# Two dense expert layers behind clustered attention: the first layer by seven block products, with block sums on GpSimd and VectorE

## The chip, the cores and the metric

The kernel runs on one core of a Trainium2 chip. The metric is the device time of one launch in microseconds (us), the median of several runs. PE is TensorE, DVE VectorE, ACT ScalarE, POOL GpSimd, and SP the queue that issues most DMAs.

## What is computed

Clustered attention (16 heads of 768 tokens, width 64) gives x of 1536 x 512. A first mixture of 8 experts takes each token to one expert of fixed capacity 192, chosen by a greedy global order. A second, dense mixture sends every token through all 4 experts and sums them by weights. The change is in the second:

```python
def _moe2_ref(x, domain_probs, w1, w2):          # x 1536x512, w1 4x512x1024, w2 4x1024x512
    p = domain_probs / (domain_probs.sum(-1, keepdims=True) + 1e-09)
    out = np.zeros((N, D), dtype=np.float32)
    for e in range(E):
        h = np.maximum(x @ w1[e], 0.0)
        out += p[:, e:e + 1] * (h @ w2[e])
    return out
```

## The kernel before

The program is one function with one block of instructions for each engine; semaphores set the order between them. Three stages follow one another: attention (to 313 us), the routed experts together with the search that assigns tokens (to 580.8 us), and the dense experts (to the end). All orders are written out by hand.

**Routed experts.** `products` (PE) runs hidden and output products of expert m with tokens as columns. ACT takes the hidden tiles (`hidden_1`, L700) and the results. `y_hi` (L720) rounds a result to `xs_hi` and DVE's `y_lo` (L964) writes the rest to `xs_lo`. POOL gathers rows (`expert_rows`), keeps the tokens' numbers (`keep_ids`, `ids_by_tile`), and gathers the mixing weights (`mix_rows`, L513).

**Dense experts.** A product in full precision is made of three passes in fp32r: each operand is split into a rounded part "hi" and the rest "lo", and `three` (L1286 to L1290) adds hi x hi, lo x hi and hi x lo in PSUM. The loops run over expert e (4), half i of the hidden width (2) and pairs of token chunks (2 x 2 chunks of 384 tokens), as hardware loops. A chunk's first layer is 4 hidden tiles `f`, each 4 depth blocks x 3 passes = 12 matmuls of 384 columns into bank `f` of `ps_h`; 48 a chunk. Its second layer is 3 token tiles, each 4 `f` x 3 passes = 12 matmuls of 512 columns into `ps_y`; 36 a chunk. PE does the first layer of two chunks and then their second layer. There are 16 such pairs; I call one a block.

ACT's `hidden_hi` (L695) writes relu of a tile as `h_hi`, DVE's `hidden_lo` (L958) writes `h_lo`, and DVE adds each weighted output tile to `X` (L1108). Each half's weights of 1 MB are loaded by SP (`load_a`, `load_b`), rounded by ACT (`split_hi_a`, `split_hi_b`, L687 and L691) and their rest is formed on POOL (`split_lo_a`, `split_lo_b`, L483 and L488). After the last block POOL scatters 12 row tiles to the output (L551).

The lines that set PE's work in the dense stage:

```python
for par in range(2):
    for f in range(KF):
        pe.wait_ge(h_taken, 8 * E + KF * (J0 + par) + f - 3)
        for a in range(KD):
            mm = three(ps_h[:, f, 0:HC], a_hi[i][:, a, fs], a_lo[i][:, a, fs],
                       xs_hi[:, a, cols], xs_lo[:, a, cols], a == 0, a == KD - 1)
        mm.then_inc(h_full, 1)
```

Of the kernel before, what the change touches and what calls it, by code (L numbers as in the profile page):

```python
# [12 lines left out]
P = 128  # L13
# [14 lines left out]
def clustered_attention_two_moes(nc, q, k, v, centroids, w_gate, w1, w2, domain_probs, v1, v2, out):  # L28
# [34 lines left out]
    CCH = NT // HALF  # L63
# [11 lines left out]
    with ExitStack() as ctx:  # L75
# [25 lines left out]
        X = sb("X", [P, NT, DM], F32)  # L101
# [58 lines left out]
        h_lo = sb("h_lo", [P, 2, KF, HC], F32R)  # L160

# [135 lines left out]
        xe_ps = ps_h[:, 0:2, 0:2 * CAP].rearrange("p a (c m) -> p a c m", c=2)  # L297

# [14 lines left out]
        def _(sp):  # L313
# [70 lines left out]

            sp.wait_ge(h_full, 8 * (E - 2) + 8)
            load_a(raw_a, a_in, 1, 0, 0)
            sp.wait_ge(y_full, 2 * (E - 2) + 2)
            load_b(raw_b, b_in, 1, 0, 0)
            sp.wait_ge(h_full, 8 * E)
            load_a(raw_a, a_in, 1, 0, 1)  # L390
            load_b(raw_b, b_in, 1, 0, 1)
            with sp.Fori(1, E2) as e:
                for i in range(2):
                    sp.wait_ge(alo_done[i], e)
                    load_a(raw_a, a_in, 1, e, i)
                    sp.wait_ge(blo_done[i], e)
                    load_b(raw_b, b_in, 1, e, i)
# [3 lines left out]
        def _(pool):  # L401
# [79 lines left out]
            def split_lo_a(i, c):  # L481
                pool.wait_ge(ahi_done[i], c + 1)
                g.tensor_tensor(a_lo[i][:], raw_a[i][:], a_hi[i][:].bitcast(F32),  # L483
                                ALU.subtract).then_inc(alo_done[i], 1)

            def split_lo_b(i, c):
                pool.wait_ge(bhi_done[i], c + 1)
                g.tensor_tensor(b_lo[i][:], raw_b[i][:], b_hi[i][:].bitcast(F32),  # L488
                                ALU.subtract).then_inc(blo_done[i], 1)
# [30 lines left out]
            for t in range(NT):  # L520
                pool.wait_ge(gt_full, t + 1)
                g.memset(X[:, t, :], 0.0).then_inc(y_zero, 1)
# [4 lines left out]
            ids_by_tile(0, 0, T_EARLY)  # L527
            for n in range(EARLY, E):
                expert_rows(n)
                keep_ids(n)  # L530
# [9 lines left out]
            pool.wait_ge(y_full, 2 * E)  # L540
            split_lo_b(0, 0)
            split_lo_a(1, 0)
            split_lo_b(1, 0)
            with pool.Fori(1, E2) as e:
                for i in range(2):
                    split_lo_a(i, e)
                    split_lo_b(i, e)
            for t in range(NT):

                pool.wait_ge(y_taken, 2 * E + (2 * E2 - 1) * NT + t + 1)  # L550
                g.indirect_dma_start(out, bass.IndirectOffsetOnAxis(ap=ids_all[:, t:t + 1], axis=0),  # L551
                                     X[:, t, :], None).then_inc(out_done, 16)
# [4 lines left out]
        def _(act):  # L557
# [127 lines left out]
            def split_hi_a(i, c):  # L685
                act.wait_ge(a_in[i], 16 * (c + 1))
                s.copy(a_hi[i][:], raw_a[i][:]).then_inc(ahi_done[i], 1)  # L687

            def split_hi_b(i, c):
                act.wait_ge(b_in[i], 16 * (c + 1))  # L690
                s.copy(b_hi[i][:], raw_b[i][:]).then_inc(bhi_done[i], 1)  # L691

            def hidden_hi(F, bank, dst):
                act.wait_ge(h_full, F + 1)
                s.activation(dst, ps_h[:, bank, 0:dst.shape[-1]], ACT.Relu).then_inc(hhi_done, 1)  # L695


# [20 lines left out]
            def y_hi(m, j):  # L718
                act.wait_ge(y_full, 2 * m + j + 1)
                s.copy(xs_hi[:, 2 * j:2 * j + 2, bass.ds(m * CAP, CAP)],  # L720
                       ps_y[:, j, 0:2 * CAP].rearrange("p (c m) -> p c m", c=2)).then_inc(yhi_done, 1)
# [9 lines left out]
            def results_and_rows(n):  # L731
                if n > 0:
                    y_hi(n - 1, 0)
                rows_1(n)
                if n > 0:
                    y_hi(n - 1, 1)
# [15 lines left out]
            for n in range(E - 2, E):  # L752
                results_and_rows(n)
                for j in range(2 * KF):
                    hidden_1(n, j)

            split_hi_a(0, E // 2)
            for j in range(2):
                y_hi(E - 1, j)
            split_hi_b(0, E // 2)  # L760

            act.wait_ge(y_full, 2 * E)

# [706 lines left out]
```

## Time and profile before

| what | us |
|---|---|
| median of 3 runs | 1124.15 |
| lowest, highest run | 1122.44, 1127.68 |
| the profiled execution, its own time | 1119.93 |
| its span, first to last instruction | 1118.1 |
| PE busy in the span | 1056.5 |
| dense stage, from its first matmul (580.8) to the span's end | 537.3 |

A row of a timeline is a start, a duration, the engine and line, the tiles written and read, and in brackets the idle time before it and what ended it. A row of groups has a count, the busy time, the mean of one in ns and the idle time before. PE's matmuls overlap, so their spacing is read from their starts and not from their durations.

### The profile page before, as it was taken

To read this page: it belongs to the slowest core of one execution; us is meant where nothing else is said; L and a number is where in the kernel's file an instruction comes from. 1 tells how busy PE (TensorE), PEld (TensorE's weight loads), DVE (VectorE), ACT (ScalarE), POOL (GpSimd) and SP (SyncE) were. 2 spreads that over 40 slices of the span, in tenths; PEclk is the share of its full clock that TensorE was granted. 3 is DMA by queue.
4 is the path that set the end of the run, shared out by engine and by line. 5 is a ranking of instruction groups with operands and counts; after the bars stand their busy time and mean duration, and the time that the engine had idled before them with its cause. 6 is when DMAs were issued, how large, how long until landed. Compare 5 with 4: busy or idle time off the path is not lost.

```text
span 1118.1 us, 18666 instructions
## 1 busy us (share of the span) xinstructions
PE 1056.5 (94%) x6650; PEld 965.2 (86%) x6650; DVE 500.0 (45%) x1107; ACT 432.3 (39%) x929; POOL 214.8 (19%) x210
## 2 busy tenths in 40 slices
PE   3999999999987899999999999999999999999996
PEld 3888888888876899998998999988999988899995
DVE  2888888888826445553012222222222222222222
ACT  3898888888732333335131221102122120211110
POOL 7033231323021001111422310302111030110022
PEclk9999999999996799999999999999999999999999
DMA  3333323232024444446942210201001000000011
GB/s 94 79 82 82 81 74 77 70 77 59 19 114 164 153 165 165 168 171 209 167 151 76 75 38 0 75 0 38 38 11 64 0 0 0 0 0 0 0 56 56
DMA packets 41351, 82.46 MB, mean 74 GB/s; under 512 B 4704, under 2 KB 10848, under 8 KB 41056
## 3 DMA queue, kind: packets, MB, share of 16 engines
q1 hardware_dynamic: 38608, 75.61, 22.1%
q0 software_dynamic: 2704, 6.33, 1.9%
q8 instruction: 25, 0.41, 0.2%
q14 instruction: 14, 0.11, 0.0%
HBM read 63.02 MB, written 6.32 MB: 62 GB/s over the span
## 4 chain that ended last, share of the span: by engine, by line
PE 82%; ACT 9%; issue 3%; DVE 3%; DMA 2%; POOL 1%; ACTq 0%; SPq 0%; DVEq 0%
PE ps_h L1290 8%; PE ps_h L1288 8%; PE ps_h L1289 8%; PE ps_h L1315 8%; PE ps_y L1290 8%; PE ps_y L1289 8%; PE ps_y L1288 8%; PE ps_y L1330 7%; PE ps_t L1193 4%; PE ps_s L1180 3%; ACT p_hi L622 2%; PE ps_s L1181 2%; PE ps_m L1154 2%; PE ps_o L1207 2%; PE ps_o L1208 2%
## 5 line engine op out<-in xcount | busy, mean ns | idle before, releaser
L695 ACT ACTIVATE h_hi<-ps_h 128x384 fp32r<-128x384 f32 x128 | 63.1, 493 | 337.1 <-PE ps_h L1290 337.1
L1288 PE MATMUL ps_h<-xs_hi,a_hi 128*128 x512 | 171.3, 335 | 0.0
L1290 PE MATMUL ps_h<-xs_lo,a_hi 128*128 x512 | 171.2, 334 | 0.0
L1289 PE MATMUL ps_h<-xs_hi,a_lo 128*128 x512 | 171.1, 334 | 0.0
L958 DVE SCALAR_TENSOR_TENSOR h_lo<-ps_h,h_hi 128x384 fp32r<-128x384 f32 x128 | 71.4, 558 | 195.5 <-ACT h_hi L695 195.5
L1108 DVE SCALAR_TENSOR_TENSOR X<-ps_y,mix_n,X 128x512 f32 x96 | 72.1, 751 | 189.4 <-PE ps_y L1290 189.4
L1290 PE MATMUL ps_y<-b_lo,h_hi 128*128 128x512 f32 x384 | 149.7, 390 | 0.0
L1289 PE MATMUL ps_y<-b_hi,h_lo 128*128 128x512 f32 x384 | 149.7, 390 | 0.0
L1288 PE MATMUL ps_y<-b_hi,h_hi 128*128 128x512 f32 x384 | 149.4, 389 | 0.0
L879 DVE TENSOR_TENSOR p_lo<-ps_t,p_hi 128x384 fp32r<-128x384 f32 x192 | 101.6, 549 | 21.6 <-ACT p_hi L622 21.5
L622 ACT CAST p_hi<-ps_t 128x384 fp32r<-128x384 f32 x192 | 87.1, 485 | 36.0 <-PE ps_t L1193 34.5
L870 DVE TENSOR_REDUCE neg_max<-ps_s 128x1 f32<-128x768 f32 x96 | 91.6, 954 | 18.2 <-PE ps_s L1181 18.2
L1288 PEld LDWEIGHTS ps_h<-xs_hi,a_hi 128*128 128x128 f32 x512 | 96.1, 188 | 0.6
L1289 PEld LDWEIGHTS ps_h<-xs_hi,a_lo 128*128 128x128 f32 x512 | 96.1, 188 | 0.6
L1290 PEld LDWEIGHTS ps_h<-xs_lo,a_hi 128*128 128x128 f32 x512 | 96.1, 188 | 0.0
L1193 PE MATMUL ps_t<-ident,probs 128*128 128x128 f32 x576 | 86.8, 278 | 7.3 <-DVE p_lo L879 6.1
L609 ACT ACTIVATE probs<-ps_s,neg_max 128x768 f32<-128x768 f32 x96 | 88.0, 917 | 2.8 <-DVE neg_max L870 2.8
L1290 PEld LDWEIGHTS ps_y<-b_lo,h_hi 128*128 128x128 f32 x384 | 72.1, 188 | 15.0
L1289 PEld LDWEIGHTS ps_y<-b_hi,h_lo 128*128 128x128 f32 x384 | 72.1, 188 | 14.7
L1288 PEld LDWEIGHTS ps_y<-b_hi,h_hi 128*128 128x128 f32 x384 | 72.1, 188 | 14.6
L1193 PEld LDWEIGHTS ps_t<-ident,probs 128*128 128x128 f32 x576 | 67.9, 142 | 19.4 <-issue 9.5
L1180 PE MATMUL ps_s<-kcT,qcT 80*128 80x384 f32 x192 | 74.8, 389 | 7.7 <-ACT kcT L597 6.6
(175 smaller groups left out, 1639.1 us busy)
## 6 DMA issues: line engine op xcount, KB each, us to landing
raw_a<-in_moe_w_dram SPq DMA_DIRECT2D x16, 1024.0 KB, 5.2
raw_b<-in_moe_w_dram SPq DMA_DIRECT2D x16, 1024.0 KB
odd_a<-in_moe_w_dram SPq DMA_DIRECT2D x8, 1024.0 KB, 8.5
odd_b<-in_moe_w_dram SPq DMA_DIRECT2D x8, 1024.0 KB
khhT<-kqT SPq DMA_DIRECT2D x32, 192.0 KB, 3.0
raw_k<-in_k_dram SPq DMA_DIRECT2D x16, 192.0 KB, 2.4
raw_q<-in_q_dram SPq DMA_DIRECT2D x16, 192.0 KB, 2.5
raw_v<-in_v_dram SPq DMA_DIRECT2D x16, 192.0 KB, 3.1
```

Of the source, the lines that this page charges most:

```text
L609: s.activation(probs[g % 2][:], ps_s[g % 2][:, :, 0:HC], ACT.Exp, bias=neg_max[:, g % 2:g % 2 + 1], scale=1.0, accum_out=row_sum[:, 2 * b ...
L622: s.copy(p_hi[u][:, a * HALF:(a + 1) * HALF, (g % HALF) * P:(g % HALF + 1) * P], ps_t[:, a, 0:HC].rearrange("p (c m) -> p c m", m=P)).then ...
L870: v_.tensor_reduce(neg_max[:, g % 2:g % 2 + 1], ps_s[g % 2][:, :, 0:HC], AX.XY, ALU.max, negate=True).then_inc(max_ready, 1)
L879: v_.tensor_tensor(p_lo[u][sl], ps_t[:, a, 0:HC].rearrange("p (c m) -> p c m", m=P), p_hi[u][sl].bitcast(F32), ALU.subtract).then_inc(plo_ ...
L1108: v_.scalar_tensor_tensor(out=row, in0=ps_y[:, (HALF * par + t) % 4, :], scalar=mix_n[:, bass.ds(tile, 1), bass.ds(e, 1)].rearrange("p a b ...
L1180: t_.matmul(dst, qcT[b][:, ts], kcT[b][:, cs], start=True, stop=False)
L1193: mm = t_.transpose(ps_t[:, a, c * P:(c + 1) * P], probs[g % 2][:, kt * P:(kt + 1) * P], ident[:])
L1288: t_.matmul(dst, w_hi, x_hi, start=first, stop=False)
L1289: t_.matmul(dst, w_lo, x_hi, start=False, stop=False)
L1290: return t_.matmul(dst, w_hi, x_lo, start=False, stop=last)
L1315: mm = t_.matmul(ps_h[:, H_BANK[j % 3], 0:CAP], wt[i][:, a, f * P:(f + 1) * P], xe[:, a, :], start=(a == 0), stop=(a == KD - 1))
L1330: mm = t_.matmul(ps_y[:, d // 2, (d % 2) * CAP:(d % 2 + 1) * CAP], wt[i][:, f, d * P:(d + 1) * P], h1[:, i * KF + f, :], start=(i == 0 and ...
```

## The change

The first layer of the dense experts is computed by Winograd's form of Strassen's method. The matrices are cut in two along each of three directions: the hidden width of a slice (2 x 128), the depth (2 x 256) and the tokens (2 x 384). Eight block products, each of 2 depth blocks x 3 passes = 6 matmuls of 384 columns, become seven, of sums of blocks.

- **Order.** Tokens are now outermost: two groups of 768 tokens, and for each all experts and halves, so 16 blocks `J` as before, written out with no loops. Weights are loaded once for each group, so twice. A block has two slices `s_` (`t` = 0, 1), each with seven products M1, M6, M7, M5, M2, M3, M4 into five banks (`M_BANK`), and then six output tiles in three banks.
- **Sums of weights** (`w_sums`, POOL): four operations of 256 columns per slice. ACT rounds seven blocks at once (`w_high`, 1792 columns), POOL forms the rest (`w_low`).
- **Sums of tokens** (`x_sums`, POOL): four operations of 768 columns per group. ACT rounds seven blocks (`x_high`); the rest is formed by DVE for group 0 and by POOL for group 1 (`x_low`).
- **Sums of products** (`slice_sums`, DVE): seven operations of 384 columns per slice, four of which write to PSUM. ACT first copies M1 out (`keep_first`). The relu and the rest of four hidden tiles (`slice_highs`, `d_low`) follow as before.
- The weights come in columns of 128 (`sum_weights`, two DMAs per slice) and single buffers of `b_raw`, `b_hi`, `b_lo`; before, each had two.
- Results of the routed experts are copied once as fp32 (`y_out`), so DVE's `y_lo` falls away, as does zeroing `X`. Outputs go to a tile `Y`; its first 6 tiles are scattered during block 8.

```diff
+        o_ps = [ps_y[:, 1 + k, :] for k in range(3)]
+        M_BANK = [{1: 0, 6: 1, 7: 2, 5: 3, 2: 0, 3: 1, 4: 4}, {1: 3, 6: 2, 7: 0, 5: 1, 2: 3, 3: 2, 4: 4}]
...
+            def w_sums(J, t):
+
+                a11, a12, a21, a22 = (w_sum[t][:, k] for k in (2, 3, 0, 1))
+                s1, s2, s3, s4 = (w_sum[t][:, k] for k in (4, 5, 6, 7))
+                pool.wait_ge(wsum_in[t], 32 * (J + 1))
+                g.tensor_tensor(s1, a21, a22, ALU.add).then_inc(wsum_step, 1)
+                g.tensor_tensor(s3, a11, a21, ALU.subtract).then_inc(wsum_step, 1)
...
+            for J in range(NJ):
+                b_low(J)
+                if J == 1:
+                    x_sums(1)
+                if J + 1 < NJ:
+                    for t in range(2):
+                        w_sums(J + 1, t)
+                    if J + 1 == NJ // 2:
+                        w_low(J + 1, 0)
+                        for k in range(5):
+                            x_low(1, k)
+                        w_low(J + 1, 1)
+                        for k in range(5, 7):
+                            x_low(1, k)
...
+            for J in range(NJ):
+                keep_first(2 * J)
+                b_high(J)
+                slice_highs(2 * J)
+                keep_first(2 * J + 1)
+                slice_highs(2 * J + 1)
+                if J + 1 < NJ:
+                    w_high(J + 1, 0)
+                    if J + 1 == NJ // 2:
+                        for k in range(7):
+                            x_high(1, k)
+                    w_high(J + 1, 1)
...
+                dve.wait_ge(c1_done, s_ + 1)
+                product_sum(s_, 2, c_16[t][:], at[6], c_1[t][:])
+                dve.wait_ge(sum_step, 7 * s_ + 1)
+                product_sum(s_, 3, c_167[t][:], at[7], c_16[t][:])
+                dve.wait_ge(sum_step, 7 * s_ + 2)
+                product_sum(s_, 4, at[7], at[5], c_167[t][:])
+                product_sum(s_, 4, c_165[t][:], at[5], c_16[t][:])
+                d_low(s_, 1, bank[7], 1, 1)
+                product_sum(s_, 5, at[2], at[2], c_1[t][:])
+                dve.wait_ge(sum_step, 7 * s_ + 4)
+                product_sum(s_, 6, at[3], at[3], c_165[t][:])
+                d_low(s_, 2, bank[2], 0, 0)
+                d_low(s_, 3, bank[3], 1, 0)
+                product_sum(s_, 7, at[4], c_167[t][:], at[4], ALU.subtract)
+                d_low(s_, 4, bank[4], 0, 1)
...
+                for a in range(2):
+                    mm = three(d_ps[M_BANK[t][m]], w_hi[t][:, slot - 1, a, :], w_lo[t][:, slot - 1, a, :],
+                               x_hi[:, part, a, :], x_lo[:, part, a, :], a == 0, a == 1)
+                mm.then_inc(m_full, 1)
...
+            def second_layer(J):
+
+                pe.wait_ge(blo_done, J + 1)
+                for q in range(TPB):
+                    n, ts = 1 - q // HALF, slice(q % HALF * P, (q % HALF + 1) * P)
+                    at_least(pe, o_taken, TPB * J + q - 2)
+                    for k, f in enumerate((0, 2, 3, 1)):
+                        if n == 1:
+                            pe.wait_ge(d_taken, 4 * (2 * J + f % 2) + (3, 1)[f // 2])
...
```

Two places of the written order. First DVE in the dense stage, before: the last `hidden_lo` of a pair of chunks and the first output tile (`y_full` counts PE's output tiles).

```order
L958 SCALAR_TENSOR_TENSOR h_lo<-ps_h,h_hi 128x384 [waits hhi_done]
L1106 ISA
L1108 ISA [waits y_full]
L1108 ISA
L1108 SCALAR_TENSOR_TENSOR X<-ps_y,mix_n,X 128x512
```

Now, one slice with `t` = 1 and the first output tiles (`c_11` is buffer 1 of `c_1`, `c_161` buffer 1 of `c_16`, and so on; the banks of `ps_h` are not told apart).

```order
L1184 TENSOR_TENSOR c_161<-ps_h,c_11 128x384 [waits m_full,c1_done]
L1184 TENSOR_TENSOR c_1671<-ps_h,c_161 128x384 [waits m_full,sum_step]
L1184 TENSOR_TENSOR ps_h<-ps_h,c_1671 128x384 [waits m_full,sum_step]
L1184 TENSOR_TENSOR c_1651<-ps_h,c_161 128x384 [waits m_full]
L1190 SCALAR_TENSOR_TENSOR h_lo<-ps_h,h_hi 128x384 [waits d_hi]
L1184 TENSOR_TENSOR ps_h<-ps_h,c_11 128x384 [waits m_full]
L1184 TENSOR_TENSOR ps_h<-ps_h,c_1651 128x384 [waits m_full,sum_step]
L1190 SCALAR_TENSOR_TENSOR h_lo<-ps_h,h_hi 128x384 [waits d_hi] x2
L1184 TENSOR_TENSOR ps_y<-c_1671,ps_y 128x384 [waits m_full]
L1190 SCALAR_TENSOR_TENSOR h_lo<-ps_y,h_hi 128x384 [waits d_hi]
```

Seven sums stand between and around the four `h_lo` of a slice, each behind a product of PE, and some behind one another.

Second POOL, before: the loop over the experts' weights.

```order
L483 TENSOR_TENSOR a_lo0<-raw_a0,a_hi0 128x2048 [waits ahi_done0]
L488 TENSOR_TENSOR b_lo0<-raw_b0,b_hi0 128x2048 [waits bhi_done0]
L483 TENSOR_TENSOR a_lo1<-raw_a1,a_hi1 128x2048 [waits ahi_done1]
L488 TENSOR_TENSOR b_lo1<-raw_b1,b_hi1 128x2048 [waits bhi_done1]
L544 REGISTER_ALU
L544 COMPARE_AND_BRANCH
```

Now, between block 7 and block 8, where the second group of tokens begins.

```order
L560 TENSOR_TENSOR w_sum1<-w_sum1 128x256 [waits wsum_step]
L565 TENSOR_TENSOR w_lo0<-w_sum0,w_hi0 128x1792 [waits whi_done0]
L548 TENSOR_TENSOR x_lo<-xs,x_hi 128x768 [waits xhi_done]
L548 TENSOR_TENSOR x_lo<-x_sum1,x_hi 128x768 [waits xhi_done]
L548 TENSOR_TENSOR x_lo<-xs,x_hi 128x768 [waits xhi_done]
L548 TENSOR_TENSOR x_lo<-x_sum0,x_hi 128x768 [waits xhi_done]
L548 TENSOR_TENSOR x_lo<-xs,x_hi 128x768 [waits xhi_done]
L565 TENSOR_TENSOR w_lo1<-w_sum1,w_hi1 128x1792 [waits whi_done1]
L548 TENSOR_TENSOR x_lo<-xs,x_hi 128x768 [waits xhi_done]
L548 TENSOR_TENSOR x_lo<-x_sum2,x_hi 128x768 [waits xhi_done]
L571 TENSOR_TENSOR b_lo<-b_raw,b_hi 128x2048 [waits bhi_done]
```

The rest of the weights of block 8 stands in one queue with the seven rests of the tokens.

## Rows read from the trace of the kernel before

**Rows 1.** The page, parts 1 and 2: PE's share of the span, its clock over 40 slices.
```profile
PE 1056.5 (94%) x6650; PEld 965.2 (86%) x6650; DVE 500.0 (45%) x1107; ACT 432.3 (39%) x929; POOL 214.8 (19%) x210
...
PEclk9999999999996799999999999999999999999999
```

**Rows 2.** The page, part 4: the chain that ended last, by engine.
```profile
PE 82%; ACT 9%; issue 3%; DVE 3%; DMA 2%; POOL 1%; ACTq 0%; SPq 0%; DVEq 0%
```

**Rows 3.** Windows of the dense stage: busy us of each engine, PEclk, DMA share, GB/s.
```profile
600.00:700.00 100.00, 100.00 (x510) 91.31 (x509) 26.99 (x43) 19.05 (x29) 19.27 (x5) 1.00 0.12 42
1000.00:1100.00 100.00, 100.00 (x509) 91.29 (x508) 27.53 (x43) 11.82 (x24) 6.87 (x8) 1.00 0.05 18
```

**Rows 4.** PE's timeline, first dense chunks: start, duration, line, tiles.
```profile
581.26 0.34 PE L1290 MATMUL ps_h<-xs_lo,a_hi 128*128 x1
...
597.38 0.33 PE L1290 MATMUL ps_h<-xs_lo,a_hi 128*128 x1
597.55 0.39 PE L1288 MATMUL ps_y<-b_hi,h_hi 128*128 128x512 f32 x1
...
613.91 0.33 PE L1288 MATMUL ps_h<-xs_hi,a_hi 128*128 x1
```

**Rows 5.** Groups by line and form, 640 to 1118 us: count, busy, mean ns, idle.
```profile
L1108 DVE SCALAR_TENSOR_TENSOR X<-ps_y,mix_n,X 128x512 f32 x88 | 66.1, 751 | 173.6 <-PE ps_y L1290 173.6
...
L958 DVE SCALAR_TENSOR_TENSOR h_lo<-ps_h,h_hi 128x384 fp32r<-128x384 f32 x112 | 62.5, 558 | 171.1 <-ACT h_hi L695 171.1
L695 ACT ACTIVATE h_hi<-ps_h 128x384 fp32r<-128x384 f32 x112 | 55.2, 493 | 300.5 <-PE ps_h L1290 300.5
...
L488 POOL TENSOR_TENSOR b_lo<-raw_b,b_hi 128x2048 fp32r<-128x2048 f32 x6 | 27.7, 4609 | 68.3 <-ACT b_hi L691 68.3
...
L691 ACT CAST b_hi<-raw_b 128x2048 fp32r<-128x2048 f32 x6 | 11.5, 1914 | 84.5 <-PE ps_y L1290 84.5
```

**Rows 6.** The same view of the whole run, POOL and DVE, 384 elements.
```profile
L466 POOL TENSOR_TENSOR q_rows<-raw_q,q_rows 128x384 fp32r<-128x384 f32 x16 | 16.0, 1002 | 1.3
...
L879 DVE TENSOR_TENSOR p_lo<-ps_t,p_hi 128x384 fp32r<-128x384 f32 x192 | 101.6, 549 | 21.6 <-ACT p_hi L622 21.5
```

**Rows 7.** Timelines of PE, ACT and DVE around the end of one group of products.
```profile
585.07 0.33 PE L1288 MATMUL ps_h<-xs_hi,a_hi 128*128 x1
585.25 0.33 PE L1289 MATMUL ps_h<-xs_hi,a_lo 128*128 x1
...
585.27 0.49 ACT L695 ACTIVATE h_hi<-ps_h 128x384 fp32r<-128x384 f32 x1 [1.48 <-PE ps_h L1290]
...
585.80 0.56 DVE L958 SCALAR_TENSOR_TENSOR h_lo<-ps_h,h_hi 128x384 fp32r<-128x384 f32 x1 [1.41 <-ACT h_hi L695]
```

**Rows 8.** POOL's timeline in the last routed experts.
```profile
511.00 1.07 POOL L508 DMA_DIRECT2D ids_all<-slot_token  x1 [7.56 <-DMA slot_token<-ids]
...
524.82 1.00 POOL L496 DMA_INDIRECT rows_in<-x_rows,ids  x1 [12.75 <-DVE ids L1000]
...
562.63 0.95 POOL L513 DMA_INDIRECT mix_n<-mix_rows,ids_all  x1 [0.30 <-issue]
```

**Rows 9.** ACT's timeline in the last routed expert.
```profile
570.71 0.33 ACT L700 ACTIVATE h<-ps_h 128x192 f32<-128x192 f32 x1 [0.97 <-PE ps_h L1315]
```

**Rows 10.** PE's timeline around its longest late wait, and an undisturbed stretch.
```profile
529.53 1.24 PE L1367 MATMUL ps_h<-place,slot_hot 128*96 128x2 bf16 x24 [1.36 <-ACT slot_hot L712]
530.63 5.17 PE L1330 MATMUL ps_y<-h,odd_b 128*128 128x192 f32 x20
...
570.51 10.56 PE L1330 MATMUL ps_y<-h,odd_b 128*128 128x192 f32 x64
```

**Rows 11.** A window inside that stretch, columns as in rows 3.
```profile
532.00:534.00 2.00, 2.00 (x8) 2.00 (x8) 0.00 (x0) 0.00 (x0) 0.00 (x0) 0.50 1.55 238
```

**Rows 12.** Timelines of DVE and POOL, the last rows of the run.
```profile
1109.82 0.75 DVE L1108 SCALAR_TENSOR_TENSOR X<-ps_y,mix_n,X 128x512 f32 x1 [1.97 <-PE ps_y L1290]
...
1110.85 0.97 POOL L551 DMA_INDIRECT out_dram<-X,ids_all  x1 [1.75 <-DVE X L1108]
```

More of the change, by code:

```diff
@@ L539, in _ @@
                 mix_rows(t)
[L540 to L552, printed above, removed]
+            for t in range(2):
+                w_sums(0, t)
+            for t in range(2):
+                w_low(0, t)
+            for J in range(NJ):
[3 more added lines that the diff above has]
+                if J + 1 < NJ:
+                    for t in range(2):
+                        w_sums(J + 1, t)
[6 more added lines that the diff above has]
+                            x_low(1, k)
+                    else:
+                        for t in range(2):
+                            w_low(J + 1, t)
+                if J == NJ // 2:
+                    rows_out(0)
+            rows_out(1)
             pool.wait_ge(out_done, 16 * NT)
@@ L1030, in phase @@
                         token_ids(n - 1)
-                    if i >= 3 and n > 1:
-                        y_lo(n - 2, i - 3)
                     dve.wait_ge(cnt_full, ND * n + i + 1)
@@ new lines, in _, with product_sum, d_low @@
+            for k in range(7):
+                dve.wait_ge(xhi_done, k + 1)
+                v_.tensor_tensor(x_lo[:, k], x_part(0, k), x_hi[:, k].bitcast(F32), ALU.subtract).then_inc(xlo_done, 1)
+            def product_sum(s_, last, out_, in0, in1, op=ALU.add):
+                dve.wait_ge(m_full, 7 * s_ + last)
+                v_.tensor_tensor(out_, in0, in1, op).then_inc(sum_step, 1)
+            def d_low(s_, k, bank, n, m):
+                f = 2 * m + s_ % 2
+                dve.wait_ge(d_hi, 4 * s_ + k)
+                v_.scalar_tensor_tensor(out=h_lo[:, n, f, :], in0=d_ps[bank], scalar=0.0,
+                                        in1=h_hi[:, n, f, :].bitcast(F32), op0=ALU.max,
+                                        op1=ALU.subtract).then_inc(d_taken, 1)
@@ new lines, in slice_sums @@
+            def slice_sums(s_):
+                t = s_ % 2
+                at = {m: d_ps[bank] for m, bank in M_BANK[t].items()}
+                bank = M_BANK[t]
+                dve.wait_ge(c1_done, s_ + 1)
[13 more added lines that the diff above has]
+                d_low(s_, 4, bank[4], 0, 1)
@@ L1114, in _ @@
+            dve.wait_ge(mix_in, 16 * NT)
+            for J in range(NJ):
+                for t in range(2):
+                    slice_sums(2 * J + t)
+                if J == NJ // 2:
+                    dve.wait_ge(xlo_done, 14)
+                outputs(J)
         @block.tensor
@@ L1447 @@
+            pe.wait_ge(h_taken, 8 * E)
+            pe.wait_ge(ids_ready, E)
+            pe.wait_ge(slot_ready, E)
+            for J in range(NJ):
+                first_layer(2 * J)
+                first_layer(2 * J + 1)
+                second_layer(J)
 _INS = ['q', 'k', 'v', 'centroids', 'moe_w_gate', 'moe_w1', 'moe_w2', 'moe2_domain_probs', 'moe2_w1', 'moe2_w2']
```

365 lines of the change are left out of this document (206 added, 159 removed).

## The prediction, made before the changed kernel had run

> **What bounds the kernel now.** I read the page first, then the chain, then windows. The page [rows 1] gives PE 1056.5 of 1118.1 us, at full clock in all but two of the 40 slices. The chain [rows 2] is PE's for 82% of the span. In the dense stage [rows 3] PE is busy for 100.00 us of every 100, at a granted clock of 1.00, while DVE is busy for 27, ACT for 12 to 19 and POOL for 7 to 19. So the matmuls there are the time, and what is removed from them is gained as long as nothing makes PE wait.
>
> PE's pace comes from starts in its timeline [rows 4]. Between 581.26 and 597.38 lie 93 matmuls of 384 columns: 0.1733 us each. Between 597.55 and 613.91 lie 72 of 512 columns: 16.36 us, 0.2272 us each. A block (two chunks) is 96 x 0.1733 + 16.36 = 33.0 us, and 16 of them make 528.
>
> **PE's part.** A block now has two slices of 42 matmuls of 384 columns, 84 for 96, with the same shapes and the same three passes; the second layer stays at 72. Removed are 12 x 0.1733 = 2.08 us a block, **33.3 us** in 16 blocks. A block is 14.56 + 16.36 = 30.92 us. PE gets more waits: one ahead of each product of 6 matmuls and one for each `f` of an output tile, 14 + 24 in a block where there were some 16. A met wait costs nothing that rows show: a new group of 12, with its wait, begins at 585.07 and its second matmul 0.18 us later, the usual pace [rows 7].
>
> **DVE's part.** The nearest row for a sum of PSUM and SBUF of 384 columns is the 549 ns of `p_lo` [rows 6]. Its result goes to SBUF; four of the seven sums write to PSUM, for which the trace has no row. Bounds: 0.49, what ACT takes for 384 from PSUM, and 0.75, what DVE takes for 512 columns [rows 5]. I take 0.55, since the operation and size are those of `p_lo`. A block costs DVE 14 x 0.55 + 8 x 0.558 + 6 x 0.751 = 16.7 us of 30.9 [rows 5]. The total is no limit, but the order may be, so I follow one block from its first matmul at 0. A product takes 6 x 0.1733 = 1.04 us, and its reader starts 0.2 us after its last issue (585.07 to 585.27 [rows 7]). From ACT's end to DVE's start is 0.04 us [rows 7].
>
> - Slice 0: the sum with M6 runs 2.3 to 2.8, with M7 to 3.9, the one on M5 to 4.9, `c_165` to 5.4, first `h_lo` to 6.0, the sums on M2 and M3 to 6.5 and 7.0, two `h_lo` to 8.1, the sum on M4 to 8.6, relu, last `h_lo` to 9.7.
> - Slice 1 starts on PE at 7.28. Its products go to banks freed at 5.4, 6.0, 7.6 and 8.1, and would be written from 7.3, 8.3, 9.4 and 10.4. M4's bank is free at 9.7 and wanted at 13.5. PE waits for none. DVE takes the first sum at 9.7, 0.2 late, and is back in step with PE at M5 (11.6).
> - Its third `h_lo` ends at 15.5. PE enters the second layer at 14.56 and wants it for the fourth `f` of the first tile, 9 x 0.227 later, at 16.6. **The slack is 1.1 us, the smallest in a block.** Seven DVE operations stand between M5 and that point, so each would have to be 0.16 us longer (0.71 for 0.55) before PE waits.
>
> **ACT's part.** Two copies of M1 and 8 relus of 0.49, `b_high` of 1.91 and two `w_high` of 1792 columns (1.91 x 1792/2048 = 1.67) make 10.2 us a block [rows 5]. `b_high` runs from 1.7 to 3.7, ahead of the relu due at 4.9.
>
> **POOL's part.** From 1.002 us for 384 and 4.609 for 2048 columns of two inputs [rows 5, 6] an operation costs 0.17 + 2.17 per 1000 columns: 0.72 for 256, 1.84 for 768, 4.06 for 1792. A block needs 4.6 + 8 x 0.72 + 2 x 4.06 = 18.5 us. `b_low` ends at 8.3 and is wanted at 14.6. The sums of the next weights end at 14.1. `w_high` starts when the first layer has been taken (16.5), so `w_low` ends at 22.2 and 26.3; PE wants them at 30.9 and 38.2. The DMAs behind them are due at 39, with 12 us for 0.5 MB. All hidden.
>
> **Block 8** is the exception: POOL also forms the seven rests of the second tokens. `w_low` ends at 22.3, five `x_low` at 31.5, the other `w_low` at 35.5, two more `x_low` at 37.4 and 39.2. PE would take M3 at 36.1 and waits 1.3, ends it at 38.4 and waits 0.8 more for M4: **2.1 us lost**, taken as 2.0. `x_sums(1)` in block 1 adds 7.4 us to POOL, and its `w_low` ends at 29.4, still in time.
>
> **Start and end.** `x_sums(0)` needs 4 x 1.84 = 7.4 us on POOL after 512.1, and the next gather starts at 524.8 [rows 8]. The mix gathers end at 563.6 [rows 8]; eight sums (5.8) and two `w_low` (8.1) end at about 577.6, before PE's 580.8. ACT's extra 0.8 us after each hidden tile of expert 6 fits beside 0.33 in the period of 1.30 (idle 0.97 [rows 9]), and three banks stand behind it. DVE's removed `y_lo`, POOL's removed zeroing and the first weights' rest lay in idle time: nothing. The tail, 0.76 of DVE and then the last scatter [rows 12], is unchanged.
>
> **Sum.** 1119.9 - 33.3 + 2.0 = **1088.6 us** for the profiled execution. The median of the runs stands 4.2 us above that execution's own time, so I forecast 1088.6 + 4.2, about **1092.5 us**.
>
> **Rivals.**
> - *DVE's chain is longer than its cover.* If sums cost 0.80 us, the slack is exceeded and PE loses about 0.4 us a block and some more in block 8, 8 us in all, and 25 us if they or the hand-overs cost 0.2 more: 1100 to 1117. For it: no row writes PSUM from DVE, and the chain crosses ACT three times. Against it: a full 0.75 for all seven still leaves PE free. Chance 0.12.
> - *POOL is slower than scaled.* Small operations with waits between them have no row. At 2.8 per 1000 columns block 8 loses 7.6 us in place of 2.0 and block 2 loses 0.3: 1092.5 + 5.9, about 1098. Chance 0.06. It is still faster than before.
> - *The change does not give PE fewer microseconds.* If each of the 22 added waits a block cost 0.09 us, 32 us return: 1124, no change. The pace across group boundaries [rows 7] speaks against it. Chance 0.05.
> - *The clock falls, slower than before.* After a wait of 1.36 us [rows 10] the granted clock was 0.50 in 532 to 534 [rows 11], the lower level of 1.2 GHz, and 20 matmuls took 5.17 us where 64 take 10.56 undisturbed [rows 10], 3.3 for 20: 1.9 us lost. If PE waited 0.6 us in each block behind DVE and each wait brought such a fall, 2.5 x 16 = 40 us are lost: 1092.5 + 40 = 1133. It decides from 31.3/16 = 1.96 us lost per block. Against it: with no wait there is no fall, and in the dense stage PE is otherwise full. Chance 0.07. The Trainium skill ("TensorE: Matmul & The Clock Gate", "HAM oscillation" and "A second HAM failure mode") says that a wait which recurs at every tile makes the engine pay the slow clock at every tile. By that rule the rival on DVE's chain would always turn into this one; the trace of before shows a single fall, and nothing of what short waits do once in each block.
>
> For block 8 alone such a fall adds at most 1.9 us; I take nothing, since a wait of 1.3 us there stands in a stretch of full work.
>
> **How the numbers follow.** My forecast has 0.70, the rivals 0.12, 0.06, 0.05 and 0.07. A difference of 0.5%, 5.6 us, is about what a measurement can tell from none. Faster: 0.70 + 0.12 + 0.06 = 0.88; same 0.05; slower 0.07. The range begins at 1086, the forecast without block 8's wait and with the runs' spread (1122.4 to 1127.7) below it, and ends at 1108, which takes in POOL's rival and half of the one on DVE's chain; about 2 in 10 lie outside.
>
> **What would show it.** Right: in windows of the dense stage PE stays at 100 with clock 1.00, blocks repeat every 30.9 us, matmuls with `ps_h` from x and w number 1344 in all, and PE's only waits are two for `x_lo` on POOL in block 8. DVE's busy time rises to about 54 of 100. Wrong on DVE's chain: PE waits for `h_lo` once a block, at the first output tile, and the sums' mean is above 0.7. Wrong on POOL: waits for `w_lo`, or `x_lo` rows well above 1.84. Wrong on pace: starts further apart than 0.1733 with no wait shown. Wrong on the clock: PEclk below 1.00 beyond the first stage.

## The result: 2.3% faster, with the dense stage as forecast and a wait of 4.8 us ahead of it

| | before | after |
|---|---|---|
| median of 4 runs, us | 1124.09 | 1098.53 |
| lowest, highest | 1122.44, 1127.68 | 1096.46, 1099.44 |
| the profiled execution, its span | 1119.93, 1118.1 | 1099.44, 1097.7 |
| PE busy, DVE busy in the span | 1056.5, 500.0 | 1030.1, 612.9 |
| dense stage: its first matmul, start of its last DVE row | 580.78, 1109.82 | 592.07, 1089.32 |

The ratio is 0.9766, between 0.9738 and 0.9794. The time fell by 25.6 us where about 31.6 were forecast (1124.15 - 1092.5); 1098.5 lies inside the range.

### The profile after

The page, parts 1, 2 and 4, answers to [rows 1, 2]:

```profile
PE 1030.1 (94%) x6458; PEld 938.3 (85%) x6458; DVE 612.9 (56%) x1321; ACT 506.3 (46%) x1007; POOL 460.6 (42%) x374
...
PEclk9999999999997699999899999999999999999999
...
PE 76%; ACT 9%; DVE 4%; POOL 3%; DMA 3%; issue 3%; ACTq 0%; SPq 0%; DVEq 0%; POOLq 0%
```

DVE, ACT and POOL all do more, and PE still holds the chain. Windows of the dense stage, and one of 10 us ahead of it (busy us of each engine, granted clock, DMA share, GB/s), answer to [rows 3]:

```profile
700.00:800.00 100.00, 100.00 (x501) 90.17 (x501) 50.71 (x90) 32.97 (x42) 59.05 (x34) 1.00 0.21 64
900.00:1000.00 100.00, 100.00 (x506) 90.83 (x506) 50.03 (x88) 31.61 (x41) 55.14 (x34) 1.00 0.22 69
520.00:530.00 10.00, 6.05 (x22) 6.06 (x23) 5.93 (x17) 3.41 (x10) 3.56 (x3) 0.66 0.39 124
```

In the dense stage DVE's busy time nearly doubles, POOL's trebles or more, and PE stays full at full clock. From 520 to 530, where routed experts run and the dense stage is still 60 us away, PE works 6.05 of 10 us at a mean granted clock of 0.66, a mixture of the two levels, 1.00 (2.4 GHz) and 0.50 (1.2 GHz). The waits of PE after 500 us, added up by line and releaser (total us, times, longest), name the place; the two left out add to 0.6 us:

```profile
PE ps_y L1479 <- DVEq L1080: 4.8, 1, 4.8
PE ps_h L1490 <- ACT slot_hot L839: 1.3, 1, 1.3
PE ps_h L1411 <- POOL x_lo L548: 0.8, 1, 0.8
PE ps_y L1411 <- POOL x_lo L548: 0.5, 1, 0.5
```

The two waits for `x_lo` were forecast. The first row was not: in the last search of the assignment, the one for the seventh expert chosen, PE waits 4.77 us for DVE's `run`. DVE's timeline there shows operations on 128 x 12 elements that take 1.3 to 1.8 us each:

```profile
516.62 0.23 DVE L1142 SCALAR_TENSOR_TENSOR e_b<-ps_y,found,first_e 128x8 f32<-128x8 f32 x1
516.88 1.32 DVE L1144 TENSOR_SCALAR over<-cur,found 128x12 f32<-128x12 f32 x1
518.12 0.15 DVE L1145 TENSOR_REDUCE e_top<-e_b 128x1 f32<-128x8 f32 x1
518.30 1.77 DVE L1146 TENSOR_SCALAR same<-cur,found 128x12 f32<-128x12 f32 x1
519.99 1.84 DVE L1147 SCALAR_TENSOR_TENSOR chosen_in<-pick,e_top,over 128x12 bf16<-128x12 f32 x1
521.86 1.72 DVE L1149 SCALAR_TENSOR_TENSOR chosen_in<-pick,e_top,same 128x12 bf16<-128x12 f32 x1
```

Before, the same four take 0.23 us each; the first and the last of them:

```profile
512.51 0.23 DVE L1049 TENSOR_SCALAR over<-cur,found 128x12 f32<-128x12 f32 x1
...
513.25 0.23 DVE L1054 SCALAR_TENSOR_TENSOR chosen_in<-pick,e_top,same 128x12 bf16<-128x12 f32 x1
```

POOL's timeline, after, over the same stretch:

```profile
516.34 1.82 POOL L538 TENSOR_TENSOR x_sum<-xs 128x768 f32<-128x768 f32 x1
518.24 1.80 POOL L540 TENSOR_TENSOR x_sum<-xs,x_sum 128x768 f32<-128x768 f32 x1
520.00 1.80 POOL L541 TENSOR_TENSOR xs<-xs 128x768 f32<-128x768 f32 x1
521.76 1.80 POOL L543 TENSOR_TENSOR x_sum<-x_sum,xs 128x768 f32<-128x768 f32 x1
```

These are `x_sums(0)`. Each long DVE operation ends within 0.1 us of the end of a POOL operation (516.88 + 1.32 = 518.20 beside 518.16, and so on for 520.04, 521.80 and 523.56). No semaphore stands between the two engines here. The Trainium skill says just this ("SBUF — State Buffer", "SBUF: two separate sides"): the two engines share a pair of ports, a DVE operation in a 2-port mode, or with two inputs in SBUF when the POOL operation reads SBUF, cannot run beside a POOL operation, and whichever is second is blocked for the other's whole length. The trace agrees: 1.3 to 1.8 us in place of 0.23, while `e_b`, which reads one of its two tensors from PSUM, keeps its 0.23 at 516.62 beside the first POOL operation. It holds longer than the rule says in two runs below, where a DVE operation waits for four POOL operations and not for one. (The TENSOR_REDUCE tells nothing: it falls into a gap of POOL.)

PE's timeline shows what follows the wait:

```profile
523.95 0.20 PE L1479 MATMUL ps_y<-chosen_in,before 128*128 128x24 bf16 x1 [4.77 <-DVEq L1080]
...
524.02 7.59 PE L1438 MATMUL ps_h<-xe,odd_a 128*128 128x192 f32 x28
```

The granted clock is 0.50 in every window of 1 us from 523 to 529, and 1.00 from 530 on. The same 28 matmuls took 4.80 us before:

```profile
514.70 4.80 PE L1315 MATMUL ps_h<-xe,odd_a 128*128 128x192 f32 x28
```

**Where the time is.** The dense stage takes 1089.32 - 592.07 = 497.25 us against 529.04, 31.8 less, and its forecast was 33.3 - 2.0 = 31.3 less. But it begins 11.3 us later. Of these, 4.8 are the wait and 2.8 the clock behind it (7.59 for 4.80). Another 4.4 were there by 491 us, ahead of any of this: `e_num` of the assignment starts at 487.27 before and at 491.63 after, which looks like a difference between two executions: the execution profiled before was 4.2 us under its median, and in the other eight profiles, of either kernel and its variants, that operation starts anywhere from 485.9 to 490.3. Small waits that are no longer there (0.7 for `slot_hot`, 0.4 on issue) give about 1 back.

The groups of the dense stage by shape, with their means, answer to [rows 5, 6]:

```profile
L565 POOL TENSOR_TENSOR w_lo<-w_sum,w_hi 128x1792 fp32r<-128x1792 f32 x30 | 121.2, 4061 | 54.9 <-ACT w_hi L796 54.9
L571 POOL TENSOR_TENSOR b_lo<-b_raw,b_hi 128x2048 fp32r<-128x2048 f32 x16 | 73.9, 4622 | 112.1 <-ACT b_hi L803 111.3 <-issue 0.8
...
L1225 DVE SCALAR_TENSOR_TENSOR Y<-ps_y,mix_n,Y 128x512 f32<-128x512 f32 x84 | 63.1, 751 | 144.3 <-PE ps_y L1413 144.3
L1184 DVE TENSOR_TENSOR c<-ps_h,c 128x384 f32<-128x384 f32 x96 | 53.1, 553 | 70.2 <-PE ps_h L1413 68.8 <-ACT c L809 1.4
L1184 DVE TENSOR_TENSOR ps_h<-ps_h,c 128x384 f32<-128x384 f32 x96 | 51.7, 563 | 15.6 <-PE ps_h L1413 15.5
L1190 DVE SCALAR_TENSOR_TENSOR h_lo<-ps_h,h_hi 128x384 fp32r<-128x384 f32 x96 | 51.5, 558 | 5.5
L796 ACT CAST w_hi<-w_sum 128x1792 fp32r<-128x1792 f32 x30 | 49.4, 1692 | 3.2 <-POOL w_sum L560 3.2
...
L560 POOL TENSOR_TENSOR w_sum<-w_sum 128x256 f32<-128x256 f32 x30 | 22.2, 739 | 2.4
```

Every duration that was scaled is there: 4.06 (4.06 forecast), 0.74 (0.72), 1.69 (1.67), sums 0.55 and 0.56 (0.55). And beside a POOL that works for 59 of 100 us, DVE's `Y` and `h_lo` keep the 751 and 558 of [rows 5], and POOL's `b_lo` its 4.6: these DVE operations read one of their tensors from PSUM, and no row shows them held.

### The profile page after: what moved, and what is told of

Its sections match the earlier page's. It is cut to its first block, busy times and chain, and to the rows that moved or that the text cites. A ratio compares the mean times of both kernels' runs of the same rounds, so it can differ in the third digit from the quotient of the medians.

```text
span 1097.7 us, 18087 instructions
## 1 busy us (share of the span) xinstructions
PE 1030.1 (94%) x6458; PEld 938.3 (85%) x6458; DVE 612.9 (56%) x1321; ACT 506.3 (46%) x1007; POOL 460.6 (42%) x374
## 4 chain that ended last, share of the span: by engine, by line
PE 76%; ACT 9%; DVE 4%; POOL 3%; DMA 3%; issue 3%; ACTq 0%; SPq 0%; DVEq 0%; POOLq 0%
PE ps_y L1412 8%; PE ps_y L1413 8%; PE ps_y L1411 8%; PE ps_y L1453 6%; PE ps_h L1438 6%; PE ps_h L1413 6%; PE ps_h L1411 6%; PE ps_h L1412 6%; PE ps_t L1316 4%; PE ps_s L1303 3%; ACT p_hi L721 2%; PE ps_s L1304 2%; PE ps_m L1277 2%; PE ps_o L1330 2%; PE ps_o L1331 2%
## 5 line engine op out<-in xcount | busy, mean ns | idle before, releaser
L565 POOL TENSOR_TENSOR w_lo<-w_sum,w_hi 128x1792 fp32r<-128x1792 f32 x32 | 129.1, 4056 | 54.9 <-ACT w_hi L796 54.9
L1225 DVE SCALAR_TENSOR_TENSOR Y<-ps_y,mix_n,Y 128x512 f32<-128x512 f32 x84 | 63.1, 751 | 144.3 <-PE ps_y L1413 144.3
L1411 PE MATMUL ps_h<-x_hi,w_hi 128*128 128x384 f32 x384 | 128.7, 335 | 0.8 <-POOL x_lo L548 0.8
L1413 PE MATMUL ps_h<-x_lo,w_hi 128*128 128x384 f32 x384 | 128.5, 335 | 0.0
L1412 PE MATMUL ps_h<-x_hi,w_lo 128*128 128x384 f32 x384 | 128.4, 334 | 0.0
L571 POOL TENSOR_TENSOR b_lo<-b_raw,b_hi 128x2048 fp32r<-128x2048 f32 x16 | 73.9, 4622 | 112.1 <-ACT b_hi L803 111.3
L586 POOL DMA_INDIRECT rows_in<-x_rows,ids x16 | 16.7, 1043 | 225.4 <-DVE ids L1097 213.6
L809 ACT COPY c<-ps_h 128x384 f32<-128x384 f32 x32 | 15.3, 477 | 180.1 <-PE ps_h L1413 180.1
L815 ACT ACTIVATE h_hi<-ps_h 128x384 fp32r<-128x384 f32 x96 | 47.2, 492 | 104.8 <-DVE ps_h L1184 104.7
L1184 DVE TENSOR_TENSOR c<-ps_h,c 128x384 f32<-128x384 f32 x96 | 53.1, 553 | 70.2 <-PE ps_h L1413 68.8
```

Of the source, the lines that this page charges most:

```text
L565: g.tensor_tensor(w_lo[t][:], w_sum[t][:, 1:8], w_hi[t][:].bitcast(F32), ALU.subtract).then_inc(wlo_done[t], 1)
L571: g.tensor_tensor(b_lo[:], b_raw[:], b_hi[:].bitcast(F32), ALU.subtract).then_inc(blo_done, 1)
L1411: t_.matmul(dst, w_hi, x_hi, start=first, stop=False)
L1412: t_.matmul(dst, w_lo, x_hi, start=False, stop=False)
L1413: return t_.matmul(dst, w_hi, x_lo, start=False, stop=last)
```

## The experiments

Each is compared with the kernel before, run on the same chip: 1122.68 (1117.67 to 1126.84) beside the first four, 1120.35 (1118.71 to 1121.81) beside the others.

| kernel | median, us | ratio to before | dense stage: first matmul, length |
|---|---|---|---|
| `again` | 1097.09 | 0.9783 [0.9748, 0.9818] | 588.85, 497.28 |
| `sums_later` | 1089.59 | 0.9710 [0.9681, 0.9740] | 581.08, 497.28 |
| `sums_later_x_early` | 1086.36 | 0.9696 [0.9664, 0.9727] | 579.02, 495.46 |
| `before_with_sums` | 1129.43 | 1.0064 [1.0038, 1.0089] | 590.72, 529.06 |
| `before_one_input` | 1132.34 | 1.0120 [1.0096, 1.0144] | 591.81, 529.05 |
| `w_sums_early` | 1087.00 | 0.9703 [0.9690, 0.9716] | 580.21, 495.48 |
| `one_more_sum` | 1087.72 | 0.9700 [0.9684, 0.9716] | 582.39, 495.48 |
| `three_more_sums` | 1097.36 | 0.9787 [0.9770, 0.9803] | 583.08, 503.94 |

The length is from the first dense matmul to the start of the last DVE row. It was 529.04 in the kernel before.

### The changed kernel again: `again`

No edit.

> The changed kernel once more, as a yardstick on the same chip. Both theories: 1098.5 us again, within 2 us; its first matmul of the dense stage near 592 us of the span, PE's longest late wait (4.8 us, at the slot ranks) there again, and PE spacing in blocks 30.9 us.

It came out at 1097.09. PE's wait in the assignment is there again, 4.5 us; the waits for `x_lo` are 0.8 and 0.5 as before, and the dense stage is as long to 0.03 us. The late start belongs to the kernel, not to one execution. Which operations are hit differs: POOL's sums begin at 514.76 here, and DVE's `same` takes 2.72 us, the second `chosen_in` 1.70 and `run` 1.76.

### The sums of tokens at another place: `sums_later`

```diff
-            x_sums(0)
...
             for n in range(EARLY, E):
...
                 keep_ids(n)
+                if n == EARLY:
+                    x_sums(0)
```

> x_sums(0) stands behind the gather and the ids of expert 6 instead of ahead of them, about 528 to 535.5 us, where DVE has next to nothing to do. Theory A (while a POOL operation with two SBUF inputs runs, DVE's small operations of the search that need both of its SBUF inputs wait for its end): the four DVE rows of 1.3 to 1.8 us shrink to 0.23, PE's wait of 4.8 us and the half clock behind it go, the dense stage begins 6.9 us earlier: 1091.6 us. Theory B (the dense stage begins late for other reasons, such as code that is written out or a run's own spread): 1098.5 us as before, within 1.5. If the later place of the sums delays the gather of expert 7 or the mix gathers, some of the gain is lost: up to 3 us.

It came out 7.5 us under `again` (1097.09 - 1089.59), where 6.9 had been expected. DVE's timeline in the step that had been held up:

```profile
513.54 0.23 DVE L1145 TENSOR_SCALAR over<-cur,found 128x12 f32<-128x12 f32 x1
...
513.87 0.23 DVE L1147 TENSOR_SCALAR same<-cur,found 128x12 f32<-128x12 f32 x1
514.01 0.23 DVE L1148 SCALAR_TENSOR_TENSOR chosen_in<-pick,e_top,over 128x12 bf16<-128x12 f32 x1
514.27 0.23 DVE L1150 SCALAR_TENSOR_TENSOR chosen_in<-pick,e_top,same 128x12 bf16<-128x12 f32 x1
```

All are back at 0.23. The same four POOL operations now stand at 528.79 to 536.0, each as long as before, and nobody waits for them. PE's wait of 4.8 is gone. The 28 matmuls behind it, in `again` and here:

```profile
520.47 7.69 PE L1438 MATMUL ps_h<-xe,odd_a 128*128 128x192 f32 x28
```

```profile
515.72 4.80 PE L1439 MATMUL ps_h<-xe,odd_a 128*128 128x192 f32 x28
```

That is 4.5 of wait and 2.9 of clock; 0.7 more is waited for `slot_hot` and 0.4 less for `h`, which leaves 7.1 of the 7.5. A change of place alone recovers what was missing.

### The same sums put into the kernel before: `before_with_sums`

Four subtractions of 768 columns on the tile `X`, at the place where the change has `x_sums(0)`; nothing reads their result.

```diff
+            pool.wait_ge(y_zero, NT)
+            xf = X[:].rearrange("p t d -> p (t d)")
+            for i in range(4):
+                g.tensor_tensor(xf[:, i * 768:(i + 1) * 768], xf[:, 3072:3840], xf[:, 3840:4608],
+                                ALU.subtract).then_inc(y_zero, 1)
...
-            dve.wait_ge(y_zero, NT)
+            dve.wait_ge(y_zero, NT + 4)
```

> The kernel before with four POOL subtractions of 768 fp32 columns and two SBUF inputs (zeros, on a tile that holds zeros) at the place where the change puts x_sums(0); nothing else. Theory A: DVE's pointer-scalar and two-input operations in the search become 1.3 to 1.8 us long, PE waits 4 to 5 us at the slot ranks and its clock falls: about 7 us slower than before, 1131 us. Theory B: POOL was idle there, so no change: 1124 us.

It cost 6.75 us (1129.43 - 1122.68), about the 7 expected. PE waits 6.45 us for `run`, and the 28 matmuls behind take 6.97 us for 4.80; the dense stage keeps its length. POOL's and DVE's timelines:

```profile
515.37 7.08 POOL L531 TENSOR_TENSOR X<-X 128x768 f32<-128x768 f32 x4
```

```profile
514.83 7.66 DVE L1054 TENSOR_SCALAR over<-cur,found 128x12 f32<-128x12 f32 x1
522.41 0.15 DVE L1055 TENSOR_REDUCE e_top<-e_b 128x1 f32<-128x8 f32 x1
522.59 0.23 DVE L1056 TENSOR_SCALAR same<-cur,found 128x12 f32<-128x12 f32 x1
```

DVE's `over` is held until the last of them ends (515.37 + 7.08 = 522.45 beside 514.83 + 7.66 = 522.49). In the changed kernel DVE got in at each change from one sum to the next, even between the second and the third (520.0), where the code has no wait and the profile no gap; so the lack of waits here doesn't explain the difference, and it stays open. The held operation began 0.54 before the first subtraction, while POOL still issued a DMA (514.28, 1.07 us), and was let through neither then nor at the change from one to the other. The product by seven has nothing to do with the loss: it is paid without it.

### With one input: `before_one_input`

```diff
-                g.tensor_tensor(xf[:, i * 768:(i + 1) * 768], xf[:, 3072:3840], xf[:, 3840:4608],
-                                ALU.subtract).then_inc(y_zero, 1)
+                g.tensor_scalar(xf[:, i * 1152:(i + 1) * 1152], xf[:, 4608:5760], 1.0, None,
+                                ALU.mult).then_inc(y_zero, 1)
```

The diff is to the kernel above.

> The kernel before with four POOL operations of 1152 fp32 columns that read one tensor only (zeros times 1.0) at the place of x_sums(0). If what holds DVE is POOL's pair of input streams (the two-input operations of before_with_sums), DVE's search keeps its 0.23 us rows and nothing changes: 1122.7 us. If any running POOL operation holds them, DVE waits for as long as these run (4 x 1.3 = 5 us by their columns): about 5 to 6 us slower, 1128 us.

```profile
511.53 12.46 POOL L531 TENSOR_SCALAR X<-X 128x1152 f32<-128x1152 f32 x4
```

```profile
512.06 11.96 DVE L1054 TENSOR_SCALAR over<-cur,found 128x12 f32<-128x12 f32 x1
```

The two fences are POOL's and DVE's timelines. DVE is held here too, for 11.96 us, and PE waits 10.7. So a POOL operation needs no second input to block `over`. I missed the size, 5 to 6 us: an operation took 3.1 us, not 1.3, and the kernel lost 12.0 us (1132.34 - 1120.35). Putting such work on POOL with one input doesn't help.

### Block 8's two waits taken away: `sums_later_x_early`

Two of the seven tokens' blocks are rounded and their rests formed ahead of the weights' rest. The diff is to `sums_later`, on POOL and on ACT.

```diff
+                        x_low(1, 0)
+                        x_low(1, 1)
                         w_low(J + 1, 0)
-                        for k in range(5):
+                        for k in range(2, 5):
...
                 keep_first(2 * J + 1)
+                if J + 1 == NJ // 2:
+                    x_high(1, 0)
+                    x_high(1, 1)
...
-                        for k in range(7):
+                        for k in range(2, 7):
```

> As sums_later, and for the second tokens ACT rounds two of the seven parts, and POOL forms their rests, inside block 7's first layer ahead of the weights of block 8. By the working of the prediction POOL is then 3.7 us earlier in block 8 for parts 5 and 6, and PE's two waits there (0.78 and 0.46 us in the profile) go: 1.2 us less than sums_later, 1090.4 us. Rival: the two roundings on ACT push the relus of block 7 and with them h_lo, and a wait at the first output tile of block 7 takes their place: no gain or up to 1 us more.

Both waits are gone, no wait for `h_lo` came, and the dense stage is 497.28 - 495.46 = 1.8 us shorter. (The medians differ by 3.2 us, more than the edit can be shown to give: the runs of each of these two kernels spread over 6 to 8 us.) It is worth seeing why it is 1.8 when the waits shown add to 1.24. PE's timeline after, at block 8:

```profile
844.80 0.34 PE L1413 MATMUL ps_h<-x_lo,w_hi 128*128 128x384 f32 x1
845.92 0.44 PE L1411 MATMUL ps_h<-x_hi,w_hi 128*128 128x384 f32 x1 [0.78 <-POOL x_lo L548]
846.20 0.34 PE L1412 MATMUL ps_h<-x_hi,w_lo 128*128 128x384 f32 x1
```

From start to start 1.12 us pass instead of 0.17, and 0.28 to the next. The bracket counts only from the end of the last matmul, which overlaps the next one in full work by 0.17. A wait shown as 0.78 cost 1.06, and the second, shown as 0.46, cost 0.7.

The kernel shows a new wait ahead of the dense stage:

```profile
PE ps_y L1459 <- ACT h L830: 1.7, 1, 1.7
```

In this execution PE comes to expert 7's output earlier, while ACT is held by `w_high(0, 1)`, which waits for POOL's `w_sums(0)` behind the gathers of the mixing weights.

### The first sums of weights ahead of these gathers: `w_sums_early`

```diff
+            for t in range(2):
+                w_sums(0, t)
             pool.wait_ge(ids_back[1], 16)
...
-            for t in range(2):
-                w_sums(0, t)
```

> As sums_later_x_early, and POOL forms the first two slices' weight sums while it waits for the last ids to come back (4.8 us idle), ahead of the last three mix gathers. There PE waits 1.7 us for ACT's last hidden tile of expert 7, which stands behind w_high(0, 1), which waits for those sums. Theory: that wait goes, 1.7 us less, 1084.7 us. Rival: the last mix gathers, which POOL now issues 1 us later, or a w_sum DMA that has not landed, give a new wait of the same size: no change.

The wait is gone, but the time is no better, where 1.7 us less had been expected: 0.9703 [0.9690, 0.9716] beside 0.9696 [0.9664, 0.9727]. Two rows of PE's timelines tell why. In `w_sums_early`, and in every other kernel here but one, the 20 matmuls behind a wait of 1.35 us for `slot_hot` take about 5 us:

```profile
529.65 1.24 PE L1496 MATMUL ps_h<-place,slot_hot 128*96 128x2 bf16 x24 [1.35 <-ACT slot_hot L842]
530.75 5.18 PE L1459 MATMUL ps_y<-h,odd_b 128*128 128x192 f32 x20
```

In the profiled execution of `sums_later_x_early`, after the same wait:

```profile
528.16 1.24 PE L1496 MATMUL ps_h<-place,slot_hot 128*96 128x2 bf16 x24 [1.35 <-ACT slot_hot L842]
529.26 3.50 PE L1459 MATMUL ps_y<-h,odd_b 128*128 128x192 f32 x20
```

Here the clock didn't fall (granted 1.00 from 529.3 to 532.7, against a mean of 0.67 from 530.75 to 535.9 in `w_sums_early`), and it was this gain of 1.7 us that brought PE to expert 7 early enough to meet the wait of 1.7. In an execution where the clock falls, the wait isn't there, and there is nothing for the edit to take away. So this run doesn't show what the edit would give in an execution that has the wait. I had priced a wait that only one execution had shown.

### DVE's chain made longer: `one_more_sum`, `three_more_sums`

These test the term on which the forecast had looked longest, the slack of 1.1 us on DVE. Both are `sums_later_x_early` with sums whose result nothing uses, ahead of `c_165` in every slice. Shown for three:

```diff
+                at_least(dve, junk_done, 3 * s_)
+                junk = h1[:].rearrange("p a c -> p (a c)")
+                for i in range(3):
+                    v_.tensor_tensor(junk[:, i * HC:(i + 1) * HC], at[5], c_16[t][:], ALU.add).then_inc(junk_done, 1)
                 product_sum(s_, 4, c_165[t][:], at[5], c_16[t][:])
```

> sums_later_x_early with one more DVE sum of 384 columns in every slice, between the sum on M5 and c_165 (its result is not used). By the prediction's working the third h_lo of a block's second slice comes 0.55 us later and the slack there is 1.1 us: no wait of PE in the dense stage, 1086.4 us as without it, within 2. If the slack were smaller than worked out: a wait at the fourth f of the first output tile in each of 16 blocks.

It came out at 1087.72, as expected. The dense stage has the length 495.48 for 495.46, with no wait of PE: one sum is within the slack.

> The same with three more sums in every slice. DVE then lags by 0.9 us when the M5 sum of the second slice is due, and three sums more make the third h_lo 2.5 us later: PE waits about 1.4 us in each block at the first output tile, 22 us in all: 1108 us. Rival (each such wait is followed by a stretch at half clock, 1.9 us each): 30 us more, 1138 us, slower than the kernel before, and a granted clock below 1.00 in every block.

It came out at 1097.36 where 1108 had been expected. Three sums cost 503.94 - 495.48 = 8.5 us against one, 0.53 a block. PE's waits, then a window of the dense stage (900 to 1000 reads 99.35 and 1.00 too), then DVE's timeline in the second slice of the second block:

```profile
PE ps_y L1422 <- DVE h_lo L1197: 3.5, 16, 0.2
```

```profile
700.00:800.00 100.00, 99.34 (x494) 88.63 (x494) 56.35 (x104) 29.13 (x39) 60.49 (x35) 1.00 0.22 69
```

```profile
627.22 1.48 DVE L1215 TENSOR_TENSOR h<-ps_h,c 128x384 f32<-128x384 f32 x3
628.62 0.55 DVE L1191 TENSOR_TENSOR c<-ps_h,c 128x384 f32<-128x384 f32 x1
...
630.66 1.02 DVE L1197 SCALAR_TENSOR_TENSOR h_lo<-ps_h,h_hi 128x384 fp32r<-128x384 f32 x2
```

The wait comes where the forecast had put it: once in each of the 16 blocks, for the third `h_lo`, at the fourth `f` of the first output tile. Operations without a wait between them follow each other by 0.47 us (three in 1.48), not by their 0.55. Three more make the chain 1.4 longer, so 15.5 becomes about 16.9 against 16.6, 0.3 to 0.4 late. (The trace has 17.0: the third `h_lo` ends at 631.68, in a block that starts at 614.68.) PE's starts there are 631.12 and 631.74, 0.39 above the usual 0.23, and the first matmul after it costs 0.11 more: 0.50. My expectation had the third `h_lo` 2.5 us later, from three full durations and a lag of DVE of 0.9; it came 1.5 later, the sums at 0.47 each and a lag of 0.3. And although PE waited in every block, the clock stayed at 1.00: so short a wait, sixteen times, brought no fall. What the Trainium skill says of a wait that recurs at every tile ("TensorE: Matmul & The Clock Gate", "HAM oscillation") is told there of waits of several microseconds. The prediction had carried it over to much shorter ones, and for waits of this size, once in 31 us, this run doesn't bear that out. Longer ones weren't tried here.

## Why the prediction was right in the dense stage and wrong ahead of it

The total came out 6.0 us above the forecast and inside the range, and for the largest miss that was luck: the range reached 15 us above the forecast to take in the rivals on POOL and DVE, which didn't come true, and not for what did.

- **PE's part, right.** Without block 8's waits the dense stage takes 495.46 us; 529.04 - 33.3 is 495.7. The added waits that are met cost nothing that 16 blocks show. The rival on PE's pace falls.
- **DVE's part, right.** Sums took 0.553 and 0.563 for 0.55. The third `h_lo` of the second slice ends 15.5 us after the block's start, as worked out (638.62 in the block that starts at 623.12), and the slack of 1.1 is borne out by both tests: 0.47 fits in it, and 1.5 overshoots it by about 0.4. DVE's busy time is 50 of 100, not 54, as operations back to back overlap. The rival on DVE's chain falls for this kernel, though it named the right place. What was put against it, that "a full 0.75 for all seven still leaves PE free", was wrong: followed through in the prediction's own way, sums of 0.75 put the third `h_lo` at 17.0, and PE would wait 0.4 in every block. The limit is the 0.71 that the prediction gives a few lines before. It made no difference, since the sums took 0.55.
- **POOL's and ACT's parts, right.** All durations within 3%. The rival on POOL falls.
- **Block 8, right.** Two waits for `x_lo`, on M3 and M4; they cost 1.8 for the 2.0 taken.
- **Start and end: this step failed.** "`x_sums(0)` needs 4 x 1.84 = 7.4 us on POOL after 512.1, and the next gather starts at 524.8": the numbers hold, and the cost of nothing drawn from them doesn't. I asked who waits for POOL and whether POOL had time. I didn't ask what runs on DVE in the same microseconds. There it was the last step of the assignment, for whose `run` PE waits, and four of its operations didn't run beside a POOL operation. The price was 4.5 to 4.8 of wait and 2.8 to 2.9 of clock behind it, 7.5 by `sums_later`. With it put back, the kernel is at 0.971 of before, 1091.5 us, against 1092.5 forecast. The some 210 us of `w_lo` and `w_sum` on POOL in the dense stage cost nothing there, where DVE's operations all read a tensor from PSUM. The seven `x_lo` of DVE ahead of that stage do have two inputs in SBUF; they met no POOL arithmetic, only its DMA issues, and kept 0.96 us each (552.83 to 561.59).
- **The clock rival.** It was placed in the dense stage, where no fall came. The fall that counts is ahead of it, behind the wait of 4.77 us, and it was part of the step that I had costed at nothing.
- **The sum against the median.** Adding 4.2 us to go from the profiled execution to the median was right in kind: the execution profiled before had the 4.4 us in hand already by 491 us.

## What to carry to other kernels

Work that is moved to an idle engine is hidden only if nobody else pays for its running: for GpSimd, look at VectorE in the same microseconds, and let POOL work stand beside DVE operations that read a tensor from PSUM, not beside a chain of small ones from SBUF to SBUF on which PE waits. A term costed at nothing because "the engine is idle there" deserves a look at the timelines of all engines in that window, and when such a wait shows up, moving the work by 14 us can be enough, as here (514.76 in `again`, 528.79 in `sums_later`). A wait in the bracket of a full PE cost 0.2 to 0.3 us more than it says here (1.06 for 0.78, 0.50 for 0.23), by the overlap lost and the slower first matmul.

## What was not expected of the hardware

- A running POOL operation holds small DVE operations (SBUF to SBUF with a scalar from a tile, or with two SBUF inputs) for as long as 7.66 and 11.96 us, through four POOL operations in a row in the two variants of the kernel before, and for one at a time in the changed kernel. What makes this difference no run shows. What reads a tensor from PSUM was not held (`e_b` 0.23, sums 0.55, `Y` 0.75), though a second tensor or a scalar came from SBUF. Nor was a TENSOR_SCALAR of one column with constants as scalars: `e_num` in `again` kept 0.15 us at 520.44, beside the last of `x_sums(0)` (520.18 to 521.98). Whether a TENSOR_REDUCE from SBUF would be held, no row shows.
- One input of 1152 columns took POOL 12.46/4 = 3.1 us, 2.7 ns a column, more than two inputs at 2.4 (1.84 for 768).
- The clock cost no more behind a longer wait: the same 28 matmuls took 7.69 us behind 4.53 of wait, 7.59 behind 4.77, 6.97 behind 6.45 and 6.42 behind 10.72. One execution of each doesn't show a rule.
- After the same wait of 1.35 us the clock fell in all kernels' profiled executions but one: 20 matmuls in about 5.2 us, or in 3.50. Why it didn't fall there stays open.
- The 4.4 us between two executions before 491 us, and why runs of one kernel lie up to 8 us apart (1084.61 to 1092.35), stay open as well.
